# Attention in front of a mixture of experts: queries and keys turned raw and split afterwards, keys moved between partition halves by transfers

## The reference, cut to what matters

```python
# q, k, v: (4 batches, 8 heads, 576 rows, 64 wide), float32
scores = scale * q @ k.T                      # per head, 576 x 576
thresh = scores.max(-1) - tau
scores = where(scores >= thresh, scores, -1e9)
attn = softmax(scores) ; x = attn @ v         # -> (2304, 512)
# then: top-1 of 8 experts (512 -> 1024 -> 512, relu, gate), on x
# then: MLP 512 -> 2048 -> 512 with g = h * sigmoid(1.702 h)
```

## Time and profile before

| | |
|---|---|
| median of 3 runs | 999.98 us |
| profiled execution, its own time | 1000.17 us |
| its span in the trace | 998.6 us |
| attention (16 pairs) | 0 to about 342 us |
| TensorE busy, whole span | 972.2 us, 97% |
| VectorE / ScalarE / GpSimd busy, whole span | 502.7 / 447.3 / 256.2 us |
| from 200 to 300 us, busy of each 100 us: PE, DVE, ACT, POOL | 99.52, 87.68, 79.54, 60.08 |
| mean granted TensorE clock | 0.995 |

### The profile page before, as it was taken

How to read it: one execution, slowest core, us unless ns; L and a number is a source line. 1 busy time by engine, 2 the same in 40 slices (tenths; PEclk the granted TensorE clock), 3 DMA queues, 4 the chain that set the end, 5 groups by cost and what they waited for, 6 DMA issues and landing times.

```text
span 998.6 us, 18965 instructions
## 1 busy us (share of the span) xinstructions
PE 972.2 (97%) x6508; PEld 867.1 (87%) x6509; DVE 502.7 (50%) x1142; ACT 447.3 (45%) x1013; POOL 256.2 (26%) x357
## 2 busy tenths in 40 slices
PE   5999999999999999999999999999999999999996
PEld 5778787878787799999999999989999999999995
DVE  6988788888889685212125155522223223222221
ACT  4778787878788514221124154422222222222221
POOL 5655565556565212111112100010010100100101
PEclk8999999999999999999999999999999999999999
DMA  3323222222344118511112542200100101000000
GB/s 62 73 60 72 47 60 65 66 49 61 91 103 130 38 42 255 178 42 42 42 42 79 173 159 64 64 32 1 32 32 0 56 7 32 32 0 0 32 1 32
DMA packets 106904, 61.08 MB, mean 61 GB/s; under 512 B 87373, under 2 KB 95587, under 8 KB 106851
## 3 DMA queue, kind: packets, MB, share of 16 engines
q1 hardware_dynamic: 96195, 44.36, 16.9%
q0 software_dynamic: 4160, 10.51, 3.4%
q10 hardware_dynamic: 6496, 5.54, 1.7%
HBM read 45.68 MB, written 14.70 MB: 60 GB/s over the span
## 4 chain that ended last, share of the span: by engine, by line
PE 92%; DVE 3%; issue 2%; ACT 1%; POOL 1%; DMA 0%; SPq 0%; ACTq 0%; POOLq 0%; DVEq 0%
PE s_ps L1790 20%; PE s_ps L1762 13%; PE s_ps L1628 11%; PE o_ps L1577 9%; PE pt_ps L1520 9%; PE s_ps L1563 8%; PE pt_ps L1762 6%; PE misc L1710 5%; PE o_ps L1710 5%; PE pt_ps L1534 3%; PE misc L1602 1%; PE pt_ps L1620 1%; PE misc L1594 1%; DMA qk<-in_k_dram 0%; ACT probs L1386 0%
## 5 line engine op out<-in xcount | busy, mean ns | idle before, releaser
L1279 DVE TENSOR_TENSOR g<-s_ps,sig 128x384 f32<-128x384 f32 x96 | 53.5, 557 | 277.1 <-ACT sig L1491 277.1
L1491 ACT ACTIVATE sig<-s_ps 128x384 f32<-128x384 f32 x96 | 47.2, 492 | 271.5 <-PE s_ps L1790 271.5
L1091 DVE TENSOR_SCALAR_CACHE_REDUCE scores<-s_ps,taus 128x576 f32<-128x576 f32 x144 | 117.7, 817 | 47.5 <-PE s_ps L1563 30.2
L802 DVE SCALAR_TENSOR_TENSOR probs<-scores,thresh,probs 128x576 f32<-128x576 f32 x144 | 136.6, 950 | 0.0
L1520 PE MATMUL pt_ps<-ident,probs 128*128 128x128 f32 x720 | 127.0, 278 | 3.9 <-ACT pT L1302 1.8
L1790 PE MATMUL s_ps<-yT_high,w_in_high 128*128 (+1 forms) x384 | 129.5, 337 | 0.3 <-issue 0.2
L1790 PE MATMUL s_ps<-yT_high,w_in_low 128*128 (+1 forms) x384 | 129.5, 337 | 0.0
L1790 PE MATMUL s_ps<-yT_low,w_in_high 128*128 (+1 forms) x384 | 128.9, 336 | 0.0
L757 POOL DMA_INDIRECT out_dram<-out_sb,table x18 | 17.8, 989 | 417.7 <-ACT out_sb L1466 414.7
L1386 ACT ACTIVATE probs<-scores,row_low 128x576 f32<-128x576 f32 x144 | 115.4, 801 | 7.5 <-DVE scores L1091 6.1
L1520 PEld LDWEIGHTS pt_ps<-ident,probs 128*128 128x128 f32 x720 | 83.5, 141 | 28.0 <-issue 18.4
(11 more groups left out here) (277 smaller groups left out, 2177.7 us busy)
## 6 DMA issues: line engine op xcount, KB each, us to landing
w_raw<-in_moe_w_dram SPq DMA_DIRECT2D x24, 512.0 KB, 4.6
yT_dram<-tile_yT ACTq DMA_DIRECT2D x10, 512.0 KB, 3.0
x_dram<-xs SPq DMA_DIRECT2D x32, 128.0 KB, 2.2
w_in_raw<-in_moe_w_in_dram SPq DMA_DIRECT2D x4, 1024.0 KB, 5.9
w_out_raw<-in_moe_w_out_dram SPq DMA_DIRECT2D x16, 256.0 KB, 2.6
qk<-in_k_dram SPq DMA_DIRECT2D x30, 128.0 KB, 2.4
next_yT<-yT_dram SPq DMA_DIRECT2D x5, 768.0 KB, 4.4
qk<-in_q_dram SPq DMA_DIRECT2D x16, 128.0 KB, 2.1
```

What stands on the lines that cost most here:

```text
L802: dve.scalar_tensor_tensor(out=probs[:, i % PROB_SLOTS, 0:SEQ], in0=scores[:, i % SCORE_SLOTS], scalar=thresh[:, j, u:u + 1], in1=probs[:, ...
L1091: dve.tensor_scalar(scores[:, i % SCORE_SLOTS].rearrange("p (c n) -> p c n", c=2), s_ps[i % 2][:, :, 0:HALF], taus[:, 3:4], None, ALU.mult ...
```

## The change

The raw queries and the raw keys of a tile stand side by side in `qk` (64 + 64 columns), so one transpose turns both: queries land in partitions 0 to 63 (TOP), keys in 64 to 127 (BOTTOM). TensorE has one transpose per tile in place of two. ScalarE copies the result to a new tile `qkT_raw`, mostly two tiles at once (`TURN_TILES`: in u1, u3, u4, u6 and u8). GpSimd splits afterwards, 64 partitions x 576 columns at a time: `split_keys` writes the high keys to the bottom of `k_swap` and the low keys to the bottom of `k_parts`; `split_queries` writes high and low queries to the two halves of `q_parts`. Side 1 is split in u0 (keys) and u1 (queries) of its own pair, side 0 of the next pair in u5 and u6. The upper halves of `k_parts` and `k_swap` are filled by two transfers from SBUF to SBUF that SP issues (`swap_keys`, 2 x 147 KB per side). `score` waits in u0 and u4 for GpSimd's count `parts_ready` and for these transfers (`k_swapped`). `qk` has two buffers, so loads wait for the transposes (`turned`) and no longer for the splits. SP's order per pair becomes `load_b`, `swap_keys` of side 1, `load_v`, `load_a`, `swap_keys` of the next side 0, `store_x`. The first load of the second expert matrices waits for the last split, half of the first expert's loads moves behind a swap, and two gathers of token rows on GpSimd move from u3 of pair 14 and u2 of pair 15 to u2 and u4 of pair 15. At the start VectorE and ScalarE split side 0 of pair 0 after it is turned, with one subtraction of it on GpSimd, and GpSimd splits side 1 of pair 0 ahead of its first threshold.

```diff
-        qk = put("qk", [P, U, 2, DH], at=DB * F1)
-        qk_parts = put("qk_parts", [P, U, 2, 2, DH], F32R)
+        qk = [put("qk0", [P, U, 2, DH], at=DB * F1), put("qk1", [P, U, 2, DH])]
+        qkT_raw = put("qkT_raw", [P, U * P])
...
-        qkT = [put(f"qkT{b}", [P, 2, 2 * SPAD], F32R) for b in range(2)]
+        q_parts = [put(f"q_parts{b}", [P, 2 * SPAD], F32R) for b in range(2)]
+        k_parts = [put(f"k_parts{b}", [P, 2 * SEQ], F32R) for b in range(2)]
         k_swap = [put(f"k_swap{b}", [P, 2 * SEQ], F32R) for b in range(2)]
...
+        Q_COLS = (slice(0, SEQ), slice(2 * SPAD - SEQ, 2 * SPAD))
+        K_COLS = (slice(0, SEQ), slice(SEQ, 2 * SEQ))
+        TOP, BOTTOM = slice(0, DH), slice(DH, P)
+        TURN_SLOT = [0, 1] * (TPB // 2) + [0] + [0, 1] * (TAIL // 2)
+        TURN_TILES = {1: (0, 2), 3: (2, 4), 4: (4, 5), 6: (5, 7), 8: (7, 9)}
...
+            def swap_keys(quad, j, side):
+
+                split = (quad * 2 + j) * 8 + side * 4 - 4
+                cols = K_COLS[side]
+                wait_apart(sp, parts_ready, split + 1)
+                sp.dma_start(k_parts[j][TOP, cols].bitcast(F32), k_swap[j][BOTTOM, cols].bitcast(F32)).then_inc(k_swapped[side], 16)
+                wait_apart(sp, parts_ready, split + 2)
+                sp.dma_start(k_swap[j][TOP, cols].bitcast(F32), k_parts[j][BOTTOM, cols].bitcast(F32)).then_inc(k_swapped[side], 16)
...
                 if (quad, j) == (QUADS - 1, 1):
                     sp.wait_ge(turned, UNITS)
+                    sp.wait_ge(parts_ready, PAIRS * 8 - 4)
                     sp.wait_ge(order_stored, 16)
-                    load_w2(sp.value_load(first_expert_i[0:1], min_val=0, max_val=E - 1), 0)
+                    load_w2(first_expert_of(sp), 0)
...
             def step(quad):
                 for j in range(2):
                     pair = quad * 2 + j
+                    if on(pair, 0, PAIRS - 2):
+                        load_b(quad + 1, j)
+                    if on(pair, 0, PAIRS):
+                        swap_keys(quad, j, 1)
                     if isinstance(quad, int):
                         early_part(quad, j)
+                    if isinstance(quad, int) and (quad, j) == (QUADS - 2, 1):
+                        sp.wait_ge(first_expert_ready, 1)
+                        load_w1(first_expert_of(sp), 0, range(2))
                     if on(pair, 0, PAIRS):
                         load_v(quad, j)
+                    if on(pair, 0, PAIRS - 2):
+                        load_a(quad + 1, j)
+                    if on(pair, 0, PAIRS - 1):
+                        swap_keys(quad + j, 1 - j, 0)
+                    if isinstance(quad, int) and (quad, j) == (QUADS - 2, 1):
+                        load_w1(first_expert_of(sp), 0, range(2, DB))
                     if on(pair, 2, PAIRS + 2):
                         store_x(quad - 1, j)
-                    if on(pair, 0, PAIRS - 2):
-                        load_b(quad + 1, j)
-                    if on(pair, 0, PAIRS - 3):
-                        load_a(quad + 1 + j, 1 - j)
...
+            def split_keys(pair, j, side):
+
+                cols = K_COLS[side]
+                done = pair * 8 + side * 4 - 4
                 wait_apart(pool, turned_copied, pair * U + (TPB if side == 0 else U))
-                cols = slice(side * SEQ, (side + 1) * SEQ)
-                done = pair * 4 + side * 2
-                pool.tensor_copy(k_swap[j][0:DH, cols], qkT[j][DH:P, 1, cols]).then_inc(k_swapped, 1)
-                wait_apart(pool, k_swapped, done + 1)
-                pool.tensor_copy(k_swap[j][DH:P, cols], qkT[j][0:DH, 1, cols]).then_inc(k_swapped, 1)
-                wait_apart(pool, k_swapped, done + 2)
-
+                pool.tensor_copy(k_swap[j][BOTTOM, cols], qkT_raw[BOTTOM, cols]).then_inc(parts_ready, 1)
+                wait_apart(pool, parts_ready, done + 1)
+                pool.tensor_tensor(k_parts[j][BOTTOM, cols], qkT_raw[BOTTOM, cols], k_swap[j][BOTTOM, cols].bitcast(F32),
+                                   ALU.subtract).then_inc(parts_ready, 1)
+                wait_apart(pool, parts_ready, done + 2)
+
+            def split_queries(pair, j, side):
+
+                cols, to = K_COLS[side], Q_COLS[side]
+                done = pair * 8 + side * 4 - 2
+                pool.tensor_copy(q_parts[j][TOP, to], qkT_raw[TOP, cols]).then_inc(parts_ready, 1)
+                wait_apart(pool, parts_ready, done + 1)
+                pool.tensor_tensor(q_parts[j][BOTTOM, to], qkT_raw[TOP, cols], q_parts[j][TOP, to].bitcast(F32),
+                                   ALU.subtract).then_inc(parts_ready, 1)
+                wait_apart(pool, parts_ready, done + 2)
...
-            split(0, 1)
-
-            split(1, 0)
+            pool.wait_ge(first_keys, 1)
+            pool.tensor_tensor(k_parts[0][BOTTOM, K_COLS[0]], qkT_raw[BOTTOM, K_COLS[0]],
+                               k_swap[0][BOTTOM, K_COLS[0]].bitcast(F32), ALU.subtract).then_inc(first_keys, 1)
+            split_keys(0, 0, 1)
+            split_queries(0, 0, 1)
...
-                    if u == 0 and on(pair, 0, PAIRS - 1):
-                        split(pair + 1, 1)
-                    if isinstance(quad, int) and (quad, i) == (QUADS - 1, 6):
-                        pool.wait_ge(tile_x_loaded, 32)
-                    if u == 1 and on(pair, 0, PAIRS):
+                    if u == 0 and on(pair, 1, PAIRS):
                         wait_apart(pool, thresh_ready, n + 1)
-                        swap(pair, j, 1)
-                    if u == 5 and on(pair, 0, PAIRS - 2):
-                        split(pair + 2, 0)
+                        split_keys(pair, j, 1)
+                    if u == 1 and on(pair, 1, PAIRS):
+                        wait_apart(pool, thresh_ready, n + 1)
+                        split_queries(pair, j, 1)
+                    if u == 5 and on(pair, 0, PAIRS - 1):
+                        wait_apart(pool, thresh_ready, n + 1)
+                        split_keys(pair + 1, 1 - j, 0)
                     if u == 6 and on(pair, 0, PAIRS - 1):
                         wait_apart(pool, thresh_ready, n + 1)
-                        swap(pair + 1, 1 - j, 0)
+                        split_queries(pair + 1, 1 - j, 0)
...
+                last = None
                 if with_probs:
-                    ins = act.copy(pT[:, TAIL, v * P:(v + 1) * P], pt_ps[:, TAIL])
-                if with_qk:
-                    at = slice(tu * P, (tu + 1) * P)
-                    if tu == TAIL:
-                        act.copy(qkT[tj][:, 0, TAIL * P:TAIL * P + LAST], pt_ps[:, QK_AT, 0:LAST])
-                        act.copy(qkT[tj][:, 0, U * P + LAST:(U + 1) * P], pt_ps[:, QK_AT, LAST:P])
-                        ins = act.copy(qkT[tj][:, 1, at], pt_ps[:, QK_AT + 1])
-                    else:
-                        ins = act.copy(qkT[tj][:, :, at], pt_ps[:, QK_AT:QK_AT + 2])
-                ins.then_inc(turned_copied, 1)
+                    last = act.copy(pT[:, TAIL, v * P:(v + 1) * P], pt_ps[:, TAIL])
+                if with_qk and tu in TURN_TILES:
+                    if tu in (1, TAIL):
+                        wait(act, parts_ready, pair * 8 + (0 if tu == 1 else 4))
+                    if isinstance(pair, int) and pair == 0 and tu == 1:
+                        act.wait_ge(first_queries, 2)
+                        act.wait_ge(first_keys, 2)
+                        act.wait_ge(k_swapped[0], 2 * 16)
+                    first, end = TURN_TILES[tu]
+                    last = act.copy(qkT_raw[:, first * P:end * P].rearrange("p (a n) -> p a n", n=P),
+                                    pt_ps[:, QK_AT:QK_AT + end - first])
+                if last is None:
+                    act.sem_inc(turned_copied, 1)
+                else:
+                    last.then_inc(turned_copied, 1)
...
-            def transpose(m, k, tj, tu, with_probs, with_qk, extra=None):
+            def transpose_qk(j, tile, to):
+
+                return pe.transpose(to, qk[j][:, tile].rearrange("p c d -> p (c d)"), ident[:])
...
                 if with_qk and tu in (0, TPB):
-                    wait(pe, parts_ready, ((m // U) * 2 + (0 if tu == 0 else 1)) * 2)
+                    loaded, each = (qk_a_loaded, A_LOADS) if tu == 0 else (qk_b_loaded, B_LOADS)
+                    wait(pe, loaded[1 - j], (quad + 1 + j) * each)
 
                 wait(pe, turned_copied, m)
                 if with_qk:
-                    for c in range(2):
-                        mm = pe.transpose(pt_ps[:, QK_AT + c],
-                                          qk_parts[:, tu, c].rearrange("p a d -> p (a d)").bitcast(F32), ident[:])
+                    mm = transpose_qk(1 - j, tu, pt_ps[:, QK_AT + TURN_SLOT[tu]])
...
-                if u == 0:
-                    wait(pe, k_swapped, (quad * 2 + j) * 4 + 2)
-                if u == TAIL:
-                    wait(pe, k_swapped, (quad * 2 + j) * 4 + 4)
```

(14 more changed lines are left out.)

139 lines of the change are left out of this document (61 added, 78 removed).

## The result

The changed kernel takes 1035.64 us, the median of 4 runs (1033.85 to 1037.78); the kernel before, on the same chip, 999.95. The ratio is 1.0357 (95% interval 1.0337 to 1.0378). The forecast was 1014.7, with 1024.5 as the upper end of the range: the sign is right, the size is not, +35.7 us in place of +14.7.

What follows compares the result with a forecast made beforehand. GpSimd's split chain and VectorE's blocked masks were to bound the period: 8 x 0.7 straight-line, 6 x 1.1 loop, 1.5 start and 1.0 last pair gave +14.7 us, so 1014.7 us; range 1001.5 to 1024.5.

Steps and rivals of the forecast that it cites:

- TensorE's saving, 0.60 us a period: In u1, u3, u4, u5 and u7, one transpose less each saves 0.12 us, if nothing else is late.
- The further 0.26 in u0: In u0, where ScalarE is late and loses its two-tile copy, up to 0.26 us more is saved.
- GpSimd's chain, 5.9 us: From threshold to scores, two copies and two subtractions take 5.9 us, or 6.8 in the loop with register waits.
- Two rings follow; the period is at least the longer: Side 1's ring sums to 19.7 us, side 0's to 19.1, or 20.65 in the loop; the longer bounds the period.
- VectorE held up, +2.6 us a period: GpSimd's subtractions block VectorE's masks, adding 2.6 us to 18.06: a straight-line period of 20.66, up 0.7.
- Loop, +1.1: Each hardware-loop period grows 1.1 us, bounds +0.7 and +1.5: a 20.65 us floor plus a mask hit.
- The loads that now wait for `turned` ... cost nothing: On SP, these loads go into a second buffer a pair ahead and cost nothing.
- Swaps hidden: The second swap lands 5.3 us after the threshold, before the queries' 5.9, hidden by 0.6 us.
- Start, +1.5: At pair 0, u4 waits for side 1's swapped keys, VectorE gives part back: +1.5 us, bounds -1 and +3.
- Last pairs: In the last pair the 5.9 us chain replaces 5.12 us: +1.0 with a blocked mask, bounds 0 and +2.
- transfers late: Rival: swaps taking twice 2.4 us land 1.8 us behind the queries each period, about 1030 us; chance 0.05.
- what I said would show it: Period 20.5 to 21.3 us, scores waiting for L685, mask mean at least 1.1 us, GpSimd up at least 20 us.

Runs made afterwards that it cites:

- zero_u1_twice: rounds_u1 with low parts left out (two copies of zeros each) and every query/key transpose done twice; 1016.25 us, 8.1 slower than without the doubling.
- zero_copies: Changed kernel with two GpSimd copies of zeros in place of each subtraction from pair 1 on, low parts left out of the computation; 1031.21 us.
- rounds_u1: act_rounds with ScalarE's two rounded copies of side 1 moved from u8 to behind u1's exp of the next pair; 1011.44 us.
- final_loop: rounds_u1 with the first half's gate stores in pieces of 256 rows and pair 0's side-1 swap ahead of the ids loads, hardware loop kept; 1010.77 us.
- final_unroll: final_loop with quads 1 to 3 written out in place of the hardware loop; 1004.87 us.
- after_split: Changed kernel with load_a of two pairs on issued with load_b, ahead of side 1's swap, and the first half's gate stores in two halves; 1033.43 us.
- gates_late: Changed kernel with SP's zeros store and first-half gate stores at pair 12 moved behind the loads of pair 14 and the swap; 1036.64 us.
- rounds_u1_gates: rounds_u1 with the first half's four gate stores issued one at a time by ScalarE in place of SyncE; 1020.72 us.
- after_early: Changed kernel with load_a issued early, with load_b, in pairs 12 and 13 alone; gate stores whole and at their place; 1033.77 us.
- rounds_start: rounds_u1 with after_split's order on SyncE and pair 0's side-1 swap ahead of the ids loads; 1006.5 us.
- act_rounds: Changed kernel with ScalarE in place of GpSimd making the rounded copies of keys and queries, GpSimd keeping the four subtractions; 1017.61 us.

## Why the prediction was wrong

The forecast was 21 us too low. The stall at pair 12 makes 9.3 of them, the other straight-line periods 4.5, the loop 4.1, the start 2.2 and the last pair 0.9. By the prediction's own steps:

- **TensorE's saving, 0.60 us a period: right** where nothing else is late (19.98 to 19.41, and some 0.5 by zero_u1_twice). The further 0.26 in u0 is not there.
- **GpSimd's chain, 5.9 us: right** in straight-line code (5.85 and 5.86), and the subtraction at 576 columns, 1.42 against the 1.44 that I had worked out. In the loop it is 7.2 and 7.1, where I had 6.8.
- **"Two rings follow; the period is at least the longer": this step failed** for the steady part, together with the masks being a floor of their own ("2.6 us, on 18.06: 20.66"). I closed each ring with the legs of the trace before, in which the other half had its slack. Both chains lie one behind the other on *one* ring, with VectorE's scaling between them, so the times add: 5.85 + 5.86, and VectorE's two legs, which the held-up masks lengthen by 2.2 us. The sum is 21.48, where the longest of three separate floors gave 20.7. With VectorE's legs as they were the same ring would be 19.3 us (an estimate: 5.85 + 1.88 + 2.66 + 5.86 + 3.04), so the error is not in either part but in taking the longer of the two. zero_copies shows the parts: without subtractions VectorE's legs are back and the period is 20.3; rounds_u1: with a shorter chain the masks are held up and next to nothing waits (0.2 us a period).
- **VectorE held up, +2.6 us a period: near** in straight-line code (its two legs +2.2, its busy time +3.1), wrong in the loop, where mostly the subtractions are held up and not the masks. The mask that starts 0.11 us behind a subtraction loses 1.92 - 0.81 = 1.11 us, while 1.31 us of the subtraction are left. The exclusive lock of the Trainium skill ("SBUF — State Buffer", "SBUF: two separate sides") would take the whole 1.31; the row stays the nearer price, and the rule is near.
- **Loop, +1.1: mis-sized**, +1.7 to +1.8. I had priced the register waits and a held mask, and put at nothing that a mask can hold up a subtraction: in the period from 78.15 us three of them lose 1.6 us together (1.86, 1.98 and 1.99 in place of 1.42). That this sets the period is read from the rows; no run tested it. final_loop against final_unroll shows that the loop lengthens the period by 0.9 us even where the chain is short and every subtraction takes 1.42 us; before, loop and straight-line periods were both close to 20.0. What those 0.9 us are is open: TensorE's longest wait in such a period is 0.4 us, for ScalarE.
- **"The loads that now wait for `turned` ... cost nothing": this step failed too,** and it is 9.3 us of the miss. I counted when the buffer is free and when a load would land, not what else SP has queued in pair 12. Before, loads ran a pair further ahead, and 10 us of slow transfers had no reader. after_split takes the stall away by loading earlier and spreading the stores; gates_late, rounds_u1_gates and after_early show that in those orders the next due transfer waits in its place.
- **Swaps hidden: right in the steady period** (2.3 us to land, and no wait of TensorE for them there), wrong at the start, and the most exposed transfers wherever the stores are.
- **Start, +1.5: mis-sized,** +3.7. The swap was issued at 18.46, as forecast, and u4's scores came at 21.46, as forecast; but VectorE gave nothing back, TensorE, at its lower level after 4.2 us of idleness (granted clock 0.50 from 21.46 to 25.5 us, 1.2 GHz), ran u4 and u5 slowly, so that u5 started at 23.52 where I had 22.2 to 23, and u0's scores then waited 1.37 us for L685. How much is which stays open. rounds_start takes the wait away and has V at 32.3.
- **Last pairs: mis-sized.** The last one has +1.9 where I had +1.0, and V14 to V15 has +3.9 where I had +0.7: the mask's mean there is 1.26 us (before 0.98), with two of the 1.2 us `w_low` subtractions on VectorE in either kernel, and TensorE waits 3.0 us for L685. That these subtractions delay the chain in the same way as the masks is argued from the rows; no run took them out.

Of the rivals, *transfers late* named the right resource with the wrong cause. Of what I said would show it, most came true (waits for L685, mean of the mask 1.09, 31.6 us more of GpSimd) with a period 0.1 to 0.4 us over the upper figure. That VectorE would hardly wait for TensorE held in the straight-line period (0.2 us, 1.9 before) and not in the loop (2.7 us, 1.7 before). And a score did wait for a transfer, at the start, which I had listed as a sign of being wrong. None of these signs could show that pair 12 would fail.

## What to carry to other kernels

When a change puts two chains of waits into one period, write the period as legs that follow each other all the way round, and lengthen each; a maximum over separate rings, each closed with old legs, is too low as soon as both have used up their slack. When loads lose a period of lead, or a transfer becomes due within the period, go through the whole in-order queue of the pair with the worst traffic, not of a typical one: a slow transfer that cost nothing before is then paid for in full.

## What the runs showed of the hardware

- Behind stores of four-byte rows the transfers that follow are slow for some 10 us, in whichever of the two queues they are: 15 and 21 GB/s in the windows above, where whole periods have 54 to 62 GB/s before the change and 81 to 87 after it. A store of 256 rows with one of 64 was followed by 7.8 us of stretched issues, 1152 rows by 9.8 in the changed kernel, 6.9 in act_rounds.
- GpSimd's one-input copies and VectorE's masks disturb each other too, mildly: the mask takes 1.14 us in place of 0.81, and two copies 1.81 in place of 1.40.
- A GpSimd subtraction and a VectorE mask hold each other up, and the one that starts second pays: a mask 0.11 us behind takes 1.92 us for 0.81, a subtraction 0.10 us behind 1.98 for 1.42.
- The hardware loop can be free or not: 19.96 to 20.04 us in it and 19.96 to 20.15 behind it before the change, 20.31 to 20.39 against 19.41 in final_loop and final_unroll.
